# Attention and two expert layers on one core: scatters between the quarters of the next pair, and queries and keys loaded six tokens to a row

## The reference

```python
def _attn_ref(q, k, v):                 # 4 batches, 8 heads, 576 tokens, 64 numbers a head
    scores = scale * np.matmul(q, k.transpose(0, 1, 3, 2))
    mask = block_i >= block_j            # blocks of 64 tokens
    scores = np.where(mask, scores, -1000000000.0)
    attn = exp(scores - max); attn = attn / (sum + 1e-09)
    return np.matmul(attn, v)
...
def reference(...):
    attn_out = _attn_ref(q, k, v)
    x = attn_out.transpose(0, 2, 1, 3).reshape(2304, 512)
    x = _moe_ref(x, ...)    # 8 experts, 512 to 1024 to 512, one expert a token, capacity 576
    return _moe2_ref(x, ...)   # a second such layer, added to x where x @ w_skip > 0
```

## Time and profile before

| | us |
|---|---|
| median of 3 runs | 683.83 |
| lowest, highest | 683.19, 685.59 |
| the profiled execution | 684.36 |
| its span, first to last instruction | 682.8 |
| TensorE busy in the span | 662.0 (97%) |
| VectorE busy | 371.4 (54%) |
| ScalarE busy | 290.7 (43%) |
| GpSimd busy | 195.7 (29%) |

### The profile page before, as it was taken

One profiled execution on the slowest core, in us unless ns is written; L12 is line 12 of the kernel. 1 busy time (PEld: TensorE's weight loads), 2 busy tenths in 40 slices (PEclk: granted clock), 3 DMA queues, 4 the chain that ended last, 5 costly groups with the idle time before them and its releaser, 6 DMA issues.

```text
span 682.8 us, 17206 instructions
## 1 busy us (share of the span) xinstructions
PE 662.0 (97%) x5640; PEld 580.6 (85%) x5641; DVE 371.4 (54%) x1029; ACT 290.7 (43%) x713; POOL 195.7 (29%) x329
## 2 busy tenths in 40 slices
PE   7999998998998999999999999999999999999997
PEld 6788887887887888989889988888899899899996
DVE  4777886886886663357733357433812453411144
ACT  4678775776775212244412244213321352411133
POOL 6523344235234122322223212123112122112112
PEclk9999999999999999999999999999999999999999
DMA  9866676555615147611521048893265778701101
GB/s 190 205 165 192 168 179 199 129 127 163 153 24 166 39 150 245 247 34 38 207 94 46 31 138 315 300 325 113 107 235 179 264 287 301 275 31 46 46 18 33
DMA packets 95616, 105.91 MB, mean 155 GB/s; under 512 B 63757, under 2 KB 63757, under 8 KB 95568
## 3 DMA queue, kind: packets, MB, share of 16 engines
q1 hardware_dynamic: 84608, 81.03, 38.2%
q0 software_dynamic: 8912, 22.36, 9.8%
q10 hardware_dynamic: 2048, 1.87, 0.8%
HBM read 83.44 MB, written 28.63 MB: 164 GB/s over the span
## 4 chain that ended last, share of the span: by engine, by line
PE 93%; DVE 2%; issue 2%; ACT 1%; another core or an unknown queue 0%; DVEq 0%; POOL 0%; ACTq 0%; POOLq 0%
PE ps L1551 33%; PE ps L1559 26%; PE ps L1446 7%; PE ps L1397 6%; PE ps L1421 5%; PE ps L1453 4%; PE ps L1373 3%; PE ps L1523 2%; PE ps L1387 2%; PE ps L1529 1%; PE ps L1414 1%; PE ps L1537 1%; DVE negmax L799 1%; PE ps L1364 1%; ACT probs L1217 0%
## 5 line engine op out<-in xcount | busy, mean ns | idle before, releaser
L1551 PE MATMUL ps<-xT,w 128*128 128x128 f32 x1344 | 159.6, 276 | 1.7 <-issue 1.5
L1551 PEld LDWEIGHTS ps<-xT,w 128*128 128x128 f32 x1344 | 155.0, 192 | 5.9 <-issue 3.9
L1559 PE MATMUL ps<-w_hi,hT_hi 128*128 128x512 f32 x256 | 104.7, 409 | 0.7 <-DVE hT_lo L1068 0.7
L1559 PE MATMUL ps<-w_lo,hT_hi 128*128 128x512 f32 x256 | 100.3, 392 | 0.0
L1559 PE MATMUL ps<-w_hi,hT_lo 128*128 128x512 f32 x256 | 99.7, 389 | 0.0
L1278 ACT ACTIVATE hT_hi<-ps 128x512 fp32r<-128x512 f32 x64 | 38.0, 593 | 115.9 <-PE ps L1551 114.4
L1551 PE MATMUL ps<-xT,w_last 128*128 128x128 f32 x704 | 86.3, 277 | 0.0
L1551 PEld LDWEIGHTS ps<-xT,w_last 128*128 128x128 f32 x704 | 82.3, 192 | 3.0 <-issue 2.2
L1068 DVE SCALAR_TENSOR_TENSOR hT_lo<-ps,hT_hi 128x512 fp32r<-128x512 f32 x64 | 44.2, 691 | 63.1 <-ACT hT_hi L1278 59.7
L1273 ACT ACTIVATE w_hi<-w2all 128x1024 fp32r (+1 forms) x48 | 47.0, 1046 | 62.6 <-PE ps L1559 56.7
L533 POOL DMA_INDIRECT out<-xs,idxo x32 | 37.4, 1169 | 110.1 <-DVE xs L1101 102.5
(11 more groups left out here) (200 smaller groups left out, 1026.0 us busy)
## 6 DMA issues: line engine op xcount, KB each, us to landing
w2all<-in_moe_w SPq DMA_DIRECT2D x10, 2048.0 KB, 15.1
w<-in_moe_w SPq DMA_DIRECT2D x7, 2048.0 KB, 9.5
rows<-queue POOLq DMA_DIRECT2D x36, 257.0 KB, 3.0
w2all<-in_moe_w SPq DMA_DIRECT2D x16, 512.0 KB, 4.6
w<-in_moe_w SPq DMA_DIRECT2D x12, 512.0 KB, 3.6
w_last<-in_moe_w SPq DMA_DIRECT2D x3, 2048.0 KB
qn<-in_q SPq DMA_DIRECT2D x32, 144.0 KB, 5.2
out<-pad SPq DMA_DIRECT2D x4, 1152.0 KB
```

The source lines that it names most:

```text
L1551: last = mm(hTp[j // 4][:, j % 4, :], w1s[slot][:, c, j * P:(j + 1) * P], xT[:, c, :], start=(c == 0), stop=(c == DC - 1))
L1559: last = mm(yp, h_[:, j, :].bitcast(f32r), w_[:, j, :].bitcast(f32r), start=(j + n == 0), stop=(j == FC - 1 and n == 2))
```

## The change

- The scatters of a batch are single calls (`scatter_tile`). Tile 0 stands behind the fourth quarter of pair 7 or 11 or 15, tiles 1 to 4 behind the four quarters of the pair that follows (8 or 12). For the third batch no pair follows and they stand directly behind. Token numbers are written behind the second quarter of pair 9, behind the wait for all five. There is a new wait for three landed scatters ahead of the last tile's copies of pairs 8 and 12.
- `whole` has three buffers, and ScalarE waits for the split three quarters back.
- `qk_parts` puts each quarter one step sooner from pair 2 on; those of pair 1 are packed more densely in pair 0.
- The scores of step 0 of a pair wait for all four quarters (two before), from pair 2 on.
- From pair 2 on queries and keys are loaded with six tokens in a row to a partition, a run of 1536 bytes. The transposed columns are then every sixth token; the rounding writes them in order (every sixth column, `every_sixth`) and the split reads and writes that way.
- VectorE's first maxima (`step_max(0)`) stand behind the first two splits and no longer behind four.

```diff
-    QUICK = 2
+    QUICK, WHOLES = 2, 3
...
-        if pair < QUICK:
-            ahead, behind = {(0, 0): ([(1, 0)], [(1, 1)]), (0, 1): ([], [(1, 2)]), (0, 2): ([], [(1, 3)]), (0, 3): ([], [(2, 0)]),
...
+        if pair == 0:
+            ahead, behind = {0: ([(1, 0)], [(1, 1)]), 1: ([(1, 2)], [(1, 3)]), 2: ([], [(2, 0)]), 3: ([], [(2, 1)])}[n]
+        elif (pair, n) == (1, 0):
+            ahead, behind = [(2, 2)], [(2, 3)]
         else:
-            ahead, behind = [], [(pair + 1 + n // 2, (n + 2) % 4)]
+            ahead, behind = [], [(pair + 2, n - 1) if n else (pair + 1, 3)]
...
+        def every_sixth(a, part):
+            half = part // 2
+            return a.rearrange("d (p j) -> d j p", j=XJ)[:, half * (XJ // 2):(half + 1) * (XJ // 2), :]
...
-                                     src[b, 2 * u + h, :, :].rearrange("(j p) d -> p j d", p=XP)).then_inc(done[par], 16)
+                        rows_of = rows_of.rearrange("(j p) d -> p j d", p=XP) if pair < QUICK else rows_of.rearrange("(p j) d -> p j d", p=XP)
...
-                g.tensor_tensor(lo[par][:, cols].bitcast(f32r), whole[i % 2][:, :], hi[par][:, cols], ALU.subtract).then_inc(qk_split, 1)
+                g.tensor_tensor(lo.bitcast(f32r), blocks(whole[i % WHOLES][:, :]), hi, ALU.subtract).then_inc(qk_split, 1)
...
                         if part == 2:
+                            if pair > NPAIR and pair % NPAIR == 0:
+                                pool.wait_ge(scattered, (pair // NPAIR - 2) * (NI * 16) + 3 * 16)
                             copy_qlast(pair)
-                if pair % NPAIR == NPAIR - 1 and pair > NPAIR:
-                    b = pair // NPAIR - 1
-                    scatter_batch(b)
-                    if b + 2 < B:
-                        write_tokens(b + 2)
+                        b = pair // NPAIR - 1
+                        if 0 <= b and pair % NPAIR == NPAIR - 1 and part == 3:
+                            scatter_tile(b, 0)
+                        if 1 <= b and pair % NPAIR == 0:
+                            scatter_tile(b - 1, part + 1)
+                        if 1 <= b and pair % NPAIR == 1 and part == 1 and b + 1 < B:
+                            pool.wait_ge(scattered, b * (NI * 16))
+                            write_tokens(b + 1)
+            for i in range(1, NI):
+                scatter_tile(B - 2, i)
...
-            for part in range(4):
-                split_qk(0, part)
-            step_max(0)
-            step_max(1)
+            for half in range(2):
+                for part in range(2 * half, 2 * half + 2):
+                    split_qk(0, part)
+                step_max(half)
...
-                if pair >= QUICK and i - 2 >= 4 * QUICK:
-                    act.wait_ge(qk_split, i - 1)
+                if pair >= QUICK and i - WHOLES >= 4 * QUICK:
+                    act.wait_ge(qk_split, i - WHOLES + 1)
...
-                    sc.activation(hi, whole[i % 2][:, :], ACT.Copy).then_inc(qk_rounded, 1)
+                    hi = every_sixth((qT_hi, kT_hi)[which][par][:, :], part).bitcast(f32r)
+                    sc.activation(hi, blocks(whole[i % WHOLES][:, :]), ACT.Copy).then_inc(qk_rounded, 1)
...
-                pe.wait_ge(qk_split, 4 * pair + (2 if n == 0 else 4))
+                pe.wait_ge(qk_split, 4 * pair + (2 if n == 0 and pair < QUICK else 4))
```

More of the change, by code:

```diff
@@ L616, in _ @@
                     pool.wait_ge(p.first_loaded[1], 16)
-                    scatter_batch(B - 1)
+                    for i in range(NI):
+                        scatter_tile(B - 1, i)
                 pool.wait_ge(p.rows_ready, 1)
```

30 lines of the change are left out of this document (14 added, 16 removed).

## The result

The changed kernel takes 680.41 us (median of 5 runs, 678.45 to 680.99); the kernel before, timed beside it, 683.83 (682.39 to 685.59). The ratio is 0.9944, with a 95% interval of 0.9925 to 0.9962: faster by a little over half a per cent. The forecast was 679.4, the range 675.5 to 686.0. The profiled execution spans 678.9 us, before 682.8.

What follows compares the result with a forecast made beforehand. In quiet attention stretches TensorE's own instructions set the pace. Terms -3.6 - 2.3 + 1.2 + 0.3 = -4.4 us took the profiled 684.36 to 680.0; the median being 0.5 lower, the forecast was 679.4, range 675.5 to 686.0.

Steps and rivals of the forecast that it cites:

- The two stops go, -5.9: Behind the first two scatter batches: spreading scatters behind the quarters removes VectorE's stalls, -3.6 and -2.3 us; bounds 0 and -5.9.
- the reading that VectorE has run out of instructions: At all three scatter batches: VectorE stalls because its instruction packet comes late from the burst of scatters; stalls 2.23, 2.24, 1.50 us.
- What is late next there is nothing.: At the first two scatter batches: once the stalls go, only TensorE's own work sets the pace, so -3.6 and -2.3 us.
- The third batch, 0: Stall near 214 us stays, though scatters begin some 1.5 us sooner: 0, bounds -3.7 and +1.
- The start, +1.2 (0.5 to 2.2): First pair: early maxima cannot start sooner and delay splits 2 and 3; with quarters moved ahead, +1.2 us, bounds 0.5 and 2.2.
- The rounding, +0.3: ScalarE writing every sixth word: +0.1 us a rounding, costing only in eight steps with weights, +0.3 us; 3 at double.
- rival D: ScalarE's strided rounding becomes much longer than double and delays TensorE in ordinary steps: 690.9 us, chance 0.08.
- The splits: GpSimd's strided split: bounds 0 and +0.8 us, some 1.2 us by the skill's rule; fits the slack, sum unchanged.
- Loads and three buffers, 0 each: Wider query and key loads and a third whole buffer: no wait of TensorE helped by themselves, worth nothing.
- B: Stalls stay or return elsewhere because q1's loads delay VectorE's packet: 685.3 us, 682.4 if half stays; chance 0.30.
- C: The stall at the third scatter batch goes too, its scatters having begun sooner: -3.7, 675.7 us, chance 0.14.

## Why the prediction was right, and where it wasn't

**The total.** 680.41 against 679.4; the profiled execution took 680.41 as well, against 680.0. The agreement is partly luck, as the terms show.

**The two stops go, -5.9.** They went: 5.45 us by the distances of the value products. The size was right, and the place. The reason was not. The step that failed is the reading that VectorE has run out of instructions: with its instructions shifted the stops stayed, and in the unchanged kernel on the third chip the packets move in the bursts and VectorE doesn't stop. That the term came out right is luck in this: whatever the reason, spreading the scatters removed it. The rule that the prediction set against that reading, that crossing a block of instructions is mostly hidden (the Trainium skill, "Runtime: NRT & Kernel Launch", "Instruction fetch mechanics"), is what the trace bears out: packets moved, and the 2.2 us stayed. What the prediction took for one mechanism is two at the same place. In the two profiles of the result and on the first chip the latest of TensorE's signals is 1.9 to 5.1 us late in a burst where five scatters stand in a row, and at most 0.45 where they are spread. On the other two chips no signal is held up, and the stop is GpSimd's wait for landed scatters with a split queued behind it. Moving that wait alone gives the whole gain there. Across the two places it is 2.88 us (from 89.71 to 118.41 before, 90.39 to 116.21 with the wait moved: 28.70 against 25.82) and 4.00 (from 144.93 to 174.75, and 142.72 to 168.54).

**"What is late next there is nothing."** Right in the changed kernel, since it moves the wait as well. But the sentence was reached without asking what that wait cost. The prediction named "a wait for all of them behind" when it described the order table and gave it no price. Its row, 2.50 us of GpSimd idle until 107.05 with two splits behind, was there to be read.

**The third batch, 0.** In the profiled execution VectorE's stop stayed, as said (1.49 and 0.78 us), but TensorE was busy 0.34 us more in those ten microseconds and kept its clock, which the prediction had valued at 1.0 there and 0.7 in the next ten. The scatters begin 0.8 us sooner against the last value products (205.5 behind 196.91, 208.9 behind 199.51), not 1.5. Measured, the changed kernel is 2.60 us ahead at the last value products before this place (196.91 against 199.51) and 3.9 at the end of the span: 1.3 us come from here, which the sum had at nothing; at the first products of the expert layer (228.05 and 224.18) the lead is already 3.87. These 1.3 us make up for the start, which cost 1.3 more than its term. On the chips without held-up signals there is no stop at this place at all, before or after.

**The start, +1.2 (0.5 to 2.2).** The mechanism was right in each step: the maxima of step 0 at 9.00, those of step 1 past 12, TensorE waiting for the splits behind them. The term was mis-sized: 1.63 us at full clock, of which 0.9 is the maxima, 0.5 the packing and 0.2 the strided order. In the execution shown it is 2.5, because its clock was low for 6.8 us at the start (39.22 against the 38.35 of the kernel with full clock) and that of before was not. A start without the change can be as slow: in the kernel with the wait moved, also low for 6.8 us, the same products stand at 38.24. So 1.5 us of the 2.5 can be the clock's alone. The stop of 1.84 us need not bring the low clock, since the kernel with scatters in a row again has the same stop and kept its full clock. The prediction priced no clock at the start. Early maxima bring nothing in any profile, and no median shows what they cost.

**The rounding, +0.3.** A rounding took 0.29 us longer, not 0.1. That is still under the 0.77 us of slack, so rival D did not come. In the steps with a piece of weights TensorE now waits 0.47 us instead of the 0.32 of the earlier trace rows, and the quiet pairs take 0.065 more each; over the fourteen pairs from the first value products of 16 to the last it comes to 0.82 us (26.80 to 210.41, 183.61, in the changed kernel on the third chip, and 23.99 to 206.78, 182.79, with spread scatters alone there). Loads, buffer and packing also differ between those two, so that all of it is the rounding isn't shown; if it is, the term was too small by 0.5.

**The splits.** On the rule of the Trainium skill for GpSimd's strides ("GPSIMD Engine Reference", "Performance pitfalls for Q7 kernels") the prediction estimated 1.2 us for a strided split; the trace has 0.956, against 0.802 in plain order. The step of 24 bytes costs a fifth more here, not a half, and TensorE hardly waited for it: 0.3 us in the whole execution.

**Loads and three buffers, 0 each.** Right: the kernel with its loads put back is no different, and the spread kernel with two buffers is faster than the changed one.

**The rivals.** B, that the stops stay because of the loads, is refuted by the kernel that has the wide loads and the stops. C's gain came in part (1.3 of 3.7 us): TensorE kept its clock, while the signals of that batch were as late as before (2.90 us). D did not come.

**What stays open.** What holds the signals up isn't shown, nor whether it goes with the chip or with the time of the runs; the records say only that they are late while the packets of scatters in a row move. The kernel with the wait moved and the scatters in a row ran only where nothing is held up, so whether it is also the best on the first chip is not known. There its row of five would be expected to hold signals up again, and spreading might still be needed. The medians on the third chip differ by 8.6 us between the kernel before and that one, the profiled executions by 6.1 (680.4 and 674.3); the profiled execution of before was the fastest of its twelve. That the others lose more through the low clock behind each stop would fit, but isn't shown.

**A faster version.** With 675.5 and 676.1 us the kernel before with only the wait moved, or only the scatters spread, beats both kernels: 1.2 to 1.4% under before, 0.2 to 0.3% under the changed kernel on the same chip.

## What to carry to other kernels

When an engine issues DMAs and then waits for their landing to reuse a buffer, look at what is queued behind that wait: move the wait to just ahead of the first instruction that needs it, before thinking about the DMAs themselves. A stop that the profile puts down to "remote" is not thereby one of instruction fetch; compare when the releasing instruction ended with when its signal was recorded. Such a stop can also cover a second one behind it; take a second execution, if possible on another chip, before naming its cause. Putting consumers "sooner" on an engine that was idle ahead of them anyway only delays the producer behind them.

## What the runs showed of the hardware

- TensorE's signals came 1.9 to 5.1 us after the end of their instructions in bursts of five indirect scatters in a row, in six profiles (four of one chip, two whose chip isn't recorded), and 0.25 to 0.45 in the six bursts of three of these profiles that have splits between the scatters. In eight profiles on two other chips they were 0.03 late at most, with the same medians of the kernel before on all three (684.3 to 684.6 us).
- ScalarE writing 288 words a partition with a step of 24 bytes took 736 ns, in plain order 443; GpSimd reading one input and writing its output so took 956 against 802.
- TensorE's clock at the start differs between executions: in the profile of before, and of the kernel with scatters in a row again, no low stretch was recorded near 10 us; in the changed kernel it was low for 6.8 us from within a stop of 1.84, and in the kernel with scatters in a row again the same stop left it at full. The profile can also show full clock where none was recorded: in the changed kernel's second profile it says 1.00 from 0 to 10 us, but the first record begins at 17.9, and the first score products have the slow pace (0.58 us for two of 256 columns, 0.39 in the first profile).
